# The inversion of the routing slots by pairs of token columns

## The chip, the cores and the metric

The kernel runs on one core of a Trainium2 chip. The core has five engines that work side by side: TensorE (matrix products, PE in the rows, with its weight loads as PEld), VectorE (DVE), ScalarE (ACT), GpSimd (POOL) and SyncE (SP, which here issues transfers). They meet by semaphores. The metric is the time on the device in microseconds. A difference of about 0.2% is what a comparison of two such kernels can tell from none.

## The reference

Three stages follow one another: a recurrent attention, a feed-forward layer with a leaky activation, and a layer of eight experts in which each expert takes exactly N / E = 384 of the N = 3072 tokens.

```python
def _moe2_ref(x, w_gate, w1, w2):
    cap = N // E
    logits = x @ w_gate
    order = np.argsort(-logits.flatten())
    for idx in order:                      # tokens go to their best expert that has room
        tok, e = idx // E, idx % E
        if assigned[tok] >= 0 or counts[e] >= cap:
            continue
        assigned[tok] = e
        counts[e] += 1
    for e in range(E):
        mask = assigned == e
        out[mask] = np.maximum(x[mask] @ w1[e], 0.0) @ w2[e]
```

## The kernel before

Attention and the first layer fill the time up to about 540 us. What matters here is the rest: eight rounds, one for each expert in the order in which the experts fill up. A round p has a routing part, which finds the expert that fills next and the 384 tokens it gets, and a feed-forward part (two layers, 384 -> 1024 -> 384, each fp32 product made of three fp32r products, `product3`). The routing of round p runs beside the feed-forward part of round p - 1, except in round 0, where nothing runs beside it.

The tokens lie on 128 partitions in NT = 24 columns. The routing part of a round is a chain between VectorE and TensorE:

- a search with six steps: VectorE makes a grid (`grid`, bf16), TensorE counts it (`count_pair`: two token columns at a time, so 12 products of 128 stationary and 16 moving columns), VectorE compares, TensorE turns the result into a digit;
- `close`, `slots`: which tokens belong to the expert, and a slot number from 1 to 384 for each (0 for the others);
- the inversion: from "token has slot s" to "slot s holds token t". VectorE splits the slot into `place` (64 values) and `col` (6 values), and marks them: `is_b` is 128 x 24 x 64 (fp16, 1 where the place fits; made in two halves of 12 columns, `inversion_b`), and `is_ar` is 128 x 24 x 6 (the token's row number where the column fits). TensorE (`inverse`) sums over all tokens: 24 products, one for each token column j, with `is_b[:, j]` (64 columns) stationary and `is_ar[:, j]` (6 columns) moving, all into 64 x 6 values of `banks[7]`. Each half has 12 of them;
- `indices`: VectorE adds N / 2 and writes the row numbers as integers to `idx`, two operations of 64 x 3. GpSimd's gather waits for them (`xg`, three indirect copies a round), TensorE transposes the gathered rows (`turn_rows`), ScalarE and VectorE split them (`xeh`, `xel`).

Where TensorE does the routing's products inside the stream of the feed-forward part is written out by hand in `body(new)`: a body has 48 places, at each stands one triple of large products (three of 128 x 384), and tables say at which place a count, a digit, the offsets, a half of the inversion or a transpose goes in ahead of the triple. The two halves of the inversion stand at places 44 and 45 (round 1), 40 and 41 (round 2), 38 and 39 (rounds 3 to 6), 25 and 26 (round 7). In round 0 they follow one another. What stands in the stream between two triples is called a break below.

VectorE's order is written out too (`route`): after `inversion_b` come `relu_lo(p - 1, 3)` (the low part of a hidden tile of the expert before, `gl` in the rows), `front_best` (the best logit of each token for the next round, ending with the `onehot` of 128 x 192), `indices`, `front_rank`, `relu_lo(p - 1, 4)`, the keys, `survivors`, and the first grid of the next round.

Of the kernel before, what the change touches and what calls it, by code (L numbers as in the profile page):

```python
# [13 lines left out]
ALU = mybir.AluOpType  # L14
# [3 lines left out]
P = 128  # L18
HALF = 64
# [13 lines left out]
def build(nc, rT, kT, rN, kN, v, wT, uR, w_in, w_out, alpha, w_gate, w1, w2, out):  # L33
# [3 lines left out]
    E, _, F2 = w1.shape  # L37
    KD = DM // P
    NF, NF2 = F // P, F2 // P
    NT = NCH * B  # L40
    N = NT * P
    CAP = N // E
    NA = CAP // P
    NS = CAP // HALF
# [5 lines left out]
    with ExitStack() as ctx:  # L50
        def sb(name, shape, dt=F32, scope=ctx):
            return scope.enter_context(nc.sbuf_tensor(name, shape, dt))

        def sem(name):
            return ctx.enter_context(nc.semaphore(name))

        banks = [ctx.enter_context(nc.psum_tensor(f"bank{i}", [P, 512], F32)) for i in range(8)]
# [54 lines left out]
        q = sb("q", [P, 2, TB], F32, one)  # L112
# [18 lines left out]
        is_b = sb("is_b", [P, NT, HALF], FP16)  # L131
        is_a = sb("is_a", [P, NT, NS])
        is_ar = sb("is_ar", [P, NT, NS], FP16)
# [30 lines left out]
        idx = sb("idx", [P, E, NA], I32)  # L164
        xeh = sb("xeh", [P, 2, KD, CAP], F32R)
        xel = sb("xel", [P, 2, KD, CAP], F32R)
        last_gh = sb("last_gh", [P, CAP], F32R)
        last_gl = sb("last_gl", [P, CAP], F32R)


        consts_loaded, u_loaded, wcol_set = sem("consts_loaded"), sem("u_loaded"), sem("wcol_set")
# [27 lines left out]
        expert_ready, idx_ready = sem("expert_ready"), sem("idx_ready")  # L199
# [35 lines left out]
        def halves(j):  # L235

            return slice(j * HALF, j * HALF + HALF)
# [560 lines left out]
        def _(dve):  # L798
# [134 lines left out]
            V = nc.vector  # L933
# [215 lines left out]
            def indices(p):  # L1149

                dve.wait_ge(inverse_done, p + 1)
                parts = banks[7][0:HALF, 0:NS].rearrange("p (a u) -> p u a", u=2)
                for u in range(2):
                    V.tensor_scalar(idx[halves(u), p], parts[:, u], float(N // 2), None, ALU.add).then_inc(idx_ready, 1)

            def while_counting(p, m):

# [135 lines left out]
            inversion_b(E - 1)  # L1293
            relu_lo(E - 2, 0)
            indices(E - 1)
            for f in range(1, 6):
                relu_lo(E - 2, f)
# [9 lines left out]
        def _(pe):  # L1307
# [151 lines left out]
            def busy(n, bank):  # L1459
                for _ in range(n):  # L1460
                    nc.tensor.matmul(bank[:, 0:TB], idle_b[:, 0:P], idle_b[:], start=True, stop=True, skip_group_check=True)
# [4 lines left out]
            for h in range(H):  # L1466
                for j in range(2):
                    mm = nc.tensor.matmul(banks[7][halves(j), h * D:(h + 1) * D], down[0:D, h], ident[0:D, 0:D],
                                          start=(h == 0), stop=(h == H - 1), skip_group_check=True)
# [38 lines left out]
            def count(p, m):  # L1508
                if m == 1:
                    pe.wait_ge(onehot_ready, p + 1)  # L1510
                if p > 0:
                    pe.wait_ge(grid_ready, 2 * V3 * (p + 1) + m)
                elif m == 1:
                    pe.wait_ge(grid_ready, 2)
                for i in range(KNOWN // 2 if p == 0 and m == 1 else 0, NT // 2):
                    if p == 0 and m > 1 and i % (NT // 4) == 0:
                        pe.wait_ge(grid_ready, 2 * m - (1 if i == 0 else 0))
                    mm = count_pair(i)
                mm.then_inc(counts_done, 1)
# [11 lines left out]
            for b in range(B):  # L1531
                for k in range(KD):
                    mm = nc.tensor.matmul(banks[7][:, b * E:(b + 1) * E], x2T[:, k, b * P:(b + 1) * P], wg[:, k],
                                          start=(b == 0 and k == 0), stop=(b == B - 1 and k == KD - 1), skip_group_check=True)
# [14 lines left out]
            def digit(p, m):  # L1549
                level, n = divmod(m - 1, V3)  # L1550
                pe.wait_ge(hits_ready, p * 2 * V3 + m)
                nc.tensor.matmul(full_at[level], sized[0:BASE_ROW + 1, level, n], hits[0:BASE_ROW + 1], start=(n == 0), stop=True, skip_group_check=True).then_inc(digit_ready, 1)

            def offsets(p):
                pe.wait_ge(running_ready, p + 1)
                nc.tensor.matmul(banks[5][:, 0:2], before_b[:], running[:].rearrange("p (s j) -> p s j", s=2)[:, :, NT - 1], start=True, stop=False, skip_group_check=True)
                nc.tensor.matmul(banks[5][:, 1:2], after_b[:], running[:, NT - 1:NT], start=False, stop=True, skip_group_check=True).then_inc(offsets_done, 1)

            def inverse(p, half):
                pe.wait_ge(inverse_ready, 3 * p + 1 + half)  # L1560
                if p == 0 and half == 0:
                    pe.wait_ge(rows_numbered, 1)
                for j in range(half * NT // 2, (half + 1) * NT // 2):
                    mm = nc.tensor.matmul(banks[7][0:HALF, 0:NS], is_b[:, j], is_ar[:, j], start=(j == 0), stop=(j == NT - 1))  # L1564
                if half == 1:
                    mm.then_inc(inverse_done, 1)

            def turn_rows(p, a):

                pe.wait_ge(gathered[a], 16 * (p + 1))  # L1570
                if a > 0 and p >= 1:
                    pe.wait_ge(xgl_ready, NA * p + a)
                for k in range(KD):
                    mm = nc.tensor.transpose(turned_rows(p, a)[:, k], xg[:, a, k * P:(k + 1) * P], ident)
                mm.then_inc(xgt_done, 1)
# [25 lines left out]
            def stream(s):  # L1601

                p, at = divmod(s, 6 * NF2)
                pair, which = divmod(at, 3)
                if pair == 0:
                    if p < E:
                        expert_hidden(p, 0, which)
                elif pair == 1:
                    if p >= 1:
                        expert_back(p - 1, NF2 - 1, which)  # L1610
                elif pair % 2 == 0:
                    expert_hidden(p, pair // 2, which)
                else:
                    expert_back(p, pair // 2 - 1, which)

            def body(new):

                q = new + 1
                counts_at = ((2, 5, 18, 23, 27, 31), (7, 11, 15, 19, 23, 27), (3, 7, 12, 17, 21, 25))[new] if new < 3 else (2, 7, 11, 16, 21, 25)
                digits_at = ((4, 6, 19, 24, 28, 32), (9, 13, 16, 20, 24, 28), (5, 10, 14, 18, 22, 26))[new] if new < 3 else (4, 9, 13, 17, 22, 26)  # L1620
                offsets_at = (36, 32)[new] if new < 2 else 30
                inverses_at = ((44, 45), (40, 41))[new] if new < 2 else (38, 39) if new < E - 2 else (25, 26)
                turns_at = ((4, 4, 5), (9, 11, 13), (7, 9, 11))[new] if new < 3 else (5, 7, 10)
                busy_at = {0: 9, 2: 2, 4: 4, 5: 2, 6: 1, 7: 1} if new == 0 else {}
                for at in range(6 * NF2):
                    if q < E - 1:
                        for m in range(2 * V3):
                            if at == counts_at[m]:
                                count(q, m + 1)
                            if at == digits_at[m]:  # L1630
                                digit(q, m + 1)
                        if at == offsets_at:
                            offsets(q)
                        if at in inverses_at:
                            inverse(q, inverses_at.index(at))
                    elif q == E - 1:
                        if at == 2:
                            offsets(q)
                        if at in inverses_at:
                            inverse(q, inverses_at.index(at))  # L1640
                    for a in range(NA):
                        if at == turns_at[a]:
                            turn_rows(new, a)
                    busy(busy_at.get(at, 0), banks[0])
                    while done[0] < 6 * NF2 * new + at + 1 - BEGINS:
                        stream(done[0])
                        done[0] += 1
# [4 lines left out]
            for m in range(1, 2 * V3 + 1):  # L1652
                count(0, m)
                digit(0, m)
                if m in (1, 2):
                    last_rows(m + 1)
            offsets(0)
            inverse(0, 0)
            inverse(0, 1)
            for p in range(E):  # L1660
                body(p)
# [38 lines left out]
```

## Time and profile before

| | |
|---|---|
| median of 3 runs | 809.49 us (808.98 to 809.88) |
| span of the profiled execution | 808.1 us, its only time on the page |
| TensorE busy | 770.3 us, 95% |
| VectorE busy | 500.5 us, 62% |
| GpSimd busy | 474.9 us, 59% |
| ScalarE busy | 220.1 us, 27% |

The span is the time from the first to the last instruction of one profiled execution; the runs are timed apart, without the profiler. TensorE's busy time is not a measure of its work, since products overlap. So the start of a product is the reliable number, and what one break takes is read from the starts around it.

### The profile page before, as it was taken

The numbers are of one execution on the slowest core, as the hardware profiler recorded it, in microseconds if no ns is written. First come the engines' busy times: TensorE is split into PE (matmuls) and PEld (weight loads), VectorE is DVE, ScalarE is ACT, GpSimd is POOL, SyncE is SP. The second block draws the span as 40 slices with busy tenths as digits, with TensorE's granted clock in tenths as the row PEclk, the third lists the DMA queues.
The fourth block names the chain that finished last, engine by engine and source line by source line (L and its number), as shares of the span: only waits on it lengthen the run. The fifth ranks groups of instructions, "written<-read, shape, count | busy, mean of one in ns | idle before, by whom it ended". The sixth has DMA issues, their size and how long they took to land.

```text
span 808.1 us, 15970 instructions
## 1 busy us (share of the span) xinstructions
PE 770.3 (95%) x6320; PEld 649.6 (80%) x6320; DVE 500.5 (62%) x1038; ACT 220.1 (27%) x452; POOL 474.9 (59%) x471
## 2 busy tenths in 40 slices
PE   6899999999999999999999999939999999999997
PEld 4578888888888888888888888726887988989996
DVE  8877766556655565556655334477787777776221
ACT  1233322111211121112111211204244344353451
POOL 6899985555555555555554333107477775775871
PEclk8999999999999999999999999958999999999999
DMA  7865522222221222222000000014523605517401
GB/s 213 228 197 155 150 70 70 69 69 70 67 67 63 66 67 63 64 64 67 11 11 11 11 11 10 14 54 168 186 74 144 215 20 198 171 45 272 159 11 49
DMA packets 46569, 75.17 MB, mean 93 GB/s; under 512 B 6256, under 2 KB 31856, under 8 KB 46496
## 3 DMA queue, kind: packets, MB, share of 16 engines
q1 hardware_dynamic: 37776, 56.07, 22.1%
q10 hardware_dynamic: 5584, 8.46, 3.7%
q0 software_dynamic: 3136, 9.64, 3.4%
q8 instruction: 50, 0.82, 0.5%
q14 instruction: 23, 0.19, 0.1%
HBM read 64.71 MB, written 9.44 MB: 92 GB/s over the span
## 4 chain that ended last, share of the span: by engine, by line
PE 81%; DVE 11%; POOL 2%; issue 2%; ACT 2%; DMA 1%; SPq 0%; POOLq 0%; DVEq 0%; ACTq 0%
PE bank L1312 23%; PE bank L1314 22%; PE bank L1313 21%; PE bank L1329 3%; PE bank L1363 3%; PE bank L1346 2%; DVE grid L1205 2%; PE bank L1422 2%; PE bank L1505 2%; DVE grid L1203 1%; POOL gl L493 1%; PE bank L1564 1%; DVE both L860 1%; PE bank L1382 1%; DVE xel L1120 1%
## 5 line engine op out<-in xcount | busy, mean ns | idle before, releaser
L493 POOL TENSOR_TENSOR gl<-g,gh 128x512 fp32r<-128x512 f32 x96 | 128.2, 1336 | 202.4 <-ACT gh L667 202.2
L1003 DVE TENSOR_SCALAR q<-bank,alpha_sb 128x512 f32<-128x512 f32 x96 | 71.9, 749 | 146.2 <-PE bank L1314 146.0
L667 ACT CAST gh<-g 128x512 fp32r<-128x512 f32 x96 | 59.6, 621 | 335.4 <-PE bank L1314 298.8
L1312 PE MATMUL bank<-gh,wout_h 128*128 128x512 f32 x288 | 118.7, 412 | 1.2 <-DVE vs L887 0.4
L1312 PE MATMUL bank<-xTh,win_h 128*128 128x512 f32 x288 | 113.1, 393 | 0.3 <-DVE xTl L896 0.3
L1314 PE MATMUL bank<-gh,wout_l 128*128 128x512 f32 x288 | 112.8, 392 | 0.0
L1313 PE MATMUL bank<-gl,wout_h 128*128 128x512 f32 x288 | 112.4, 390 | 0.0
L1314 PE MATMUL bank<-xTh,win_l 128*128 128x512 f32 x288 | 112.2, 389 | 0.0
L1313 PE MATMUL bank<-xTl,win_h 128*128 128x512 f32 x288 | 112.0, 389 | 0.0
L599 POOL TENSOR_TENSOR w1l<-raw,w1h 128x384 fp32r<-128x384 f32 x64 | 65.1, 1016 | 38.4 <-ACT w2h L731 37.9
L1312 PE MATMUL bank<-xeh,w1h 128*128 128x384 f32 x192 | 69.6, 362 | 0.0
L1006 DVE SCALAR_TENSOR_TENSOR g<-bank,q 128x512 f32<-128x512 f32 x96 | 66.4, 691 | 3.3
L1312 PE MATMUL bank<-w2h,gh 128*128 128x384 f32 x189 | 68.0, 360 | 0.1
L1312 PEld LDWEIGHTS bank<-gh,wout_h 128*128 128x128 f32 x288 | 54.1, 188 | 14.7 <-POOL gl L493 2.6
L600 POOL TENSOR_TENSOR w2l<-raw,w2h 128x384 fp32r<-128x384 f32 x64 | 64.9, 1015 | 0.0
L1314 PE MATMUL bank<-xeh,w1l 128*128 128x384 f32 x192 | 64.7, 337 | 0.0
L1313 PE MATMUL bank<-xel,w1h 128*128 128x384 f32 x192 | 64.4, 336 | 0.0
L1313 PE MATMUL bank<-w2l,gh 128*128 128x384 f32 x189 | 63.8, 338 | 0.0
L1314 PEld LDWEIGHTS bank<-gh,wout_l 128*128 128x128 f32 x288 | 54.0, 188 | 12.1
L1314 PE MATMUL bank<-w2h,gl 128*128 128x384 f32 x189 | 63.7, 337 | 0.0
L1312 PEld LDWEIGHTS bank<-xTh,win_h 128*128 128x128 f32 x288 | 54.1, 188 | 11.8 <-DVE xTl L896 0.8
L1314 PEld LDWEIGHTS bank<-xTh,win_l 128*128 128x128 f32 x288 | 54.1, 188 | 11.5
(203 smaller groups left out, 1453.6 us busy)
## 6 DMA issues: line engine op xcount, KB each, us to landing
raw<-w SPq DMA_DIRECT2D x32, 768.0 KB
rt<-rT SPq DMA_DIRECT2D x48, 96.0 KB, 2.9
vs<-v SPq DMA_DIRECT2D x48, 96.0 KB, 3.0
vn<-v SPq DMA_DIRECT2D x24, 192.0 KB, 2.9
x2rows<-x2n SPq DMA_DIRECT2D x23, 192.0 KB, 1.9
kt<-kT SPq DMA_DIRECT2D x44, 96.0 KB, 2.5
kn<-kN SPq DMA_DIRECT2D x20, 192.0 KB, 2.5
rn<-rN SPq DMA_DIRECT2D x20, 192.0 KB, 2.6
```

The source lines that it names most:

```text
L493: nc.gpsimd.tensor_tensor(gl[:, f % 2], g[:, f % 2], gh[:, f % 2].bitcast(F32), ALU.subtract).then_inc(gl_ready, 1)
L599: nc.gpsimd.tensor_tensor(w1l[:, f], raw1[:, p % 2, :, f * P:(f + 1) * P], w1h[:, f].bitcast(F32), ALU.subtract).then_inc(wlo1_ready, 1)
L600: nc.gpsimd.tensor_tensor(w2l[:, f], raw2[:, p % 2, f, :], w2h[:, f].bitcast(F32), ALU.subtract).then_inc(wlo_ready, 1)
L667: nc.scalar.copy(gh[:, f % 2], g[:, f % 2]).then_inc(gh_ready, 1)
L1003: nc.vector.tensor_scalar(q[:, f % 2], h, 0.0, alpha_sb[:, f:f + 1], ALU.min, ALU.mult).then_inc(q_ready, 1)
L1006: nc.vector.scalar_tensor_tensor(out=g[:, f % 2], in0=h, scalar=0.0, in1=q[:, f % 2], op0=ALU.max, op1=ALU.add).then_inc(g_ready, 1)
L1205: V.scalar_tensor_tensor(out=grid[:, js, 0:R], in0=wide, scalar=found[level], in1=row, op0=ALU.subtract, op1=ALU.is_ge).then_inc(grid_read ...
L1312: nc.tensor.matmul(o, a_h, b_h, start=first, stop=False)
L1313: nc.tensor.matmul(o, a_h, b_l, start=False, stop=False)
L1314: return nc.tensor.matmul(o, a_l, b_h, start=False, stop=last)
L1329: mm = nc.tensor.matmul(score_bank(c, b, j)[halves(j), h * HT:(h + 1) * HT], kt[heads_in(j), b % 2, h], weights(c, b)[heads_in(j), j, h], ...
L1363: return nc.tensor.matmul(y_bank(c, b)[halves(j), cols], weights(c, b)[:, j, h], vs[:, b, j, cols], start=(h == 0), stop=(h == H - 1), ski ...
```

## The change

The inversion takes two token columns at a time. The stationary operand is `is_b` of columns 2i and 2i + 1 side by side (128 columns), the moving one is `is_ar` of the same two (12 columns), and 12 products give 128 x 12 values. Of their four blocks the two diagonal ones are wanted: rows 0 to 63 with columns 0 to 5 (even token columns), and rows 64 to 127 with columns 6 to 11 (odd ones). VectorE adds N / 2 to the second and writes it to a new tile, `odd_rows`, in partitions 0 to 63, waits until that is written, and then adds the two blocks into `idx`, again in two operations. TensorE does all 12 products at one place, the later of the two; it still waits for the first half of `is_b` ahead of the first six and for the second half ahead of the others.

```diff
+        odd_rows = sb("odd_rows", [P, NS])
...
                 dve.wait_ge(inverse_done, p + 1)
-                parts = banks[7][0:HALF, 0:NS].rearrange("p (a u) -> p u a", u=2)
+                inv_hold(V.tensor_scalar(odd_rows[0:HALF], banks[7][halves(1), NS:2 * NS], float(N // 2), None, ALU.add))
+                even, odd = (a.rearrange("p (a u) -> p u a", u=2) for a in (banks[7][0:HALF, 0:NS], odd_rows[0:HALF]))
                 for u in range(2):
-                    V.tensor_scalar(idx[halves(u), p], parts[:, u], float(N // 2), None, ALU.add).then_inc(idx_ready, 1)
+                    V.tensor_tensor(idx[halves(u), p], even[:, u], odd[:, u], ALU.add).then_inc(idx_ready, 1)
...
                 pe.wait_ge(inverse_ready, 3 * p + 1 + half)
                 if p == 0 and half == 0:
                     pe.wait_ge(rows_numbered, 1)
-                for j in range(half * NT // 2, (half + 1) * NT // 2):
-                    mm = nc.tensor.matmul(banks[7][0:HALF, 0:NS], is_b[:, j], is_ar[:, j], start=(j == 0), stop=(j == NT - 1))
+                for i in range(half * NT // 4, (half + 1) * NT // 4):
+                    mm = nc.tensor.matmul(banks[7][:, 0:2 * NS], is_b[:, 2 * i:2 * i + 2].rearrange("p j s -> p (j s)"),
+                                          is_ar[:, 2 * i:2 * i + 2].rearrange("p j s -> p (j s)"), start=(i == 0), stop=(i == NT // 2 - 1))
...
-                inverses_at = ((44, 45), (40, 41))[new] if new < 2 else (38, 39) if new < E - 2 else (25, 26)
+                inverse_at = (45, 41)[new] if new < 2 else 39 if new < E - 2 else 26
...
-                        if at in inverses_at:
-                            inverse(q, inverses_at.index(at))
+                        if at == inverse_at:
+                            inverse(q, 0)
+                            inverse(q, 1)
```

On TensorE, in the stream of round 3's inversion, the order before is this (each row one product, L1564 the inversion, the others the triples):

```order
L1312 MATMUL bank<-w2h,gh 128x384
L1313 MATMUL bank<-w2l,gh 128x384
L1314 MATMUL bank<-w2h,gl 128x384
L1564 MATMUL bank<-is_ar,is_b 64x6 x12
L1312 MATMUL bank<-w2h,gh 128x384
L1313 MATMUL bank<-w2l,gh 128x384
L1314 MATMUL bank<-w2h,gl 128x384
L1564 MATMUL bank<-is_ar,is_b 64x6 x12
L1312 MATMUL bank<-xeh,w1h 128x384
L1313 MATMUL bank<-xel,w1h 128x384
L1314 MATMUL bank<-xeh,w1l 128x384
```

and at the same place of the changed kernel (its lines are numbered two higher there):

```order
L1314 MATMUL bank<-w2h,gh 128x384
L1315 MATMUL bank<-w2l,gh 128x384
L1316 MATMUL bank<-w2h,gl 128x384
L1314 MATMUL bank<-w2h,gh 128x384
L1315 MATMUL bank<-w2l,gh 128x384
L1316 MATMUL bank<-w2h,gl 128x384
L1566 MATMUL bank<-is_ar,is_b 128x12 x12
L1314 MATMUL bank<-xeh,w1h 128x384
L1315 MATMUL bank<-xel,w1h 128x384
L1316 MATMUL bank<-xeh,w1l 128x384
```

One break is gone, and the triple that stood between the two now comes ahead of both halves.

On VectorE, behind the making of `is_b` in a round from 3 on, before:

```order
L1147 TENSOR_TENSOR is_b<-iota_b,bank 128x768 x2
L1113 SCALAR_TENSOR_TENSOR gl<-bank,gh 128x384
L956 TENSOR_REDUCE bank<-logits 128x24
L957 TENSOR_TENSOR onehot<-logits,bank 128x192
L1154 TENSOR_SCALAR idx<-bank 64x3 x2
L961 TENSOR_TENSOR ranked<-onehot,bank 128x192
L962 TENSOR_REDUCE bank<-ranked 128x24
L1113 SCALAR_TENSOR_TENSOR gl<-bank,gh 128x384
L970 TENSOR_TENSOR onehot<-ranked,bank 128x192
```

and after the change (lines one or two higher):

```order
L1148 TENSOR_TENSOR is_b<-iota_b,bank 128x768 x2
L1114 SCALAR_TENSOR_TENSOR gl<-bank,gh 128x384
L957 TENSOR_REDUCE bank<-logits 128x24
L958 TENSOR_TENSOR onehot<-logits,bank 128x192
L1153 TENSOR_SCALAR odd_rows<-bank 64x6
L1156 TENSOR_TENSOR idx<-bank,odd_rows 64x3 x2
L962 TENSOR_TENSOR ranked<-onehot,bank 128x192
L963 TENSOR_REDUCE bank<-ranked 128x24
L1114 SCALAR_TENSOR_TENSOR gl<-bank,gh 128x384
L971 TENSOR_TENSOR onehot<-ranked,bank 128x192
```

The operation on `odd_rows` is new, ahead of the indices, and nothing else has moved.

## Rows read from the trace of the kernel before

**Rows 1.** The page: span, and the chain that ended last by engine.

```profile
span 808.1 us, 15970 instructions
...
PE 81%; DVE 11%; POOL 2%; issue 2%; ACT 2%; DMA 1%; SPq 0%; POOLq 0%; DVEq 0%; ACTq 0%
```

**Rows 2.** Busy: stage, us, PE, PEld, DVE, ACT, POOL, clock, DMA share, GB/s.

```profile
668.50:700.00 31.50, 31.27 (x259) 28.07 (x258) 24.41 (x71) 13.31 (x30) 21.55 (x22) 1.00 0.39 132
790.00:800.00 10.00, 10.00 (x60) 10.00 (x59) 2.23 (x4) 1.94 (x5) 0.00 (x0) 1.00 0.00 0
```

**Rows 3.** Timeline, TensorE, one old break: start us, us, engine, line, work, [idle].

```profile
636.23 0.34 PE L1314 MATMUL bank<-w2h,gl 128*128 128x384 f32 x1
...
636.49 0.45 PEld L1564 LDWEIGHTS bank<-is_ar,is_b 128*64 128x64 f16 x12 [0.25 <-DVE is_b L1147]
...
636.97 0.45 PE L1312 MATMUL bank<-w2h,gh 128*128 128x384 f32 x1
...
637.25 0.33 PE L1313 MATMUL bank<-w2l,gh 128*128 128x384 f32 x1
```

**Rows 4.** The same view, one break for a count.

```profile
643.87 0.34 PE L1314 MATMUL bank<-w2h,gl 128*128 128x384 f32 x1
...
644.04 0.37 PEld L1505 LDWEIGHTS bank<-onehot,grid 128*128 128x128 bf16 x12 [0.16 <-issue]
...
644.36 0.42 PE L1312 MATMUL bank<-w2h,gh 128*128 128x384 f32 x1
...
644.62 0.33 PE L1313 MATMUL bank<-w2l,gh 128*128 128x384 f32 x1
```

**Rows 5.** Timeline, VectorE: a small operation with a PSUM and an SBUF input.

```profile
644.74 0.16 DVE L1211 TENSOR_TENSOR hits<-bank,rest 40x8 bf16<-40x8 f32 x1
```

**Rows 6.** Timeline, VectorE, round 3: from is_b to the next grid.

```profile
635.27 1.81 DVE L1147 TENSOR_TENSOR is_b<-iota_b,bank 128x768 f16<-128x768 bf16 x2
...
637.85 0.35 DVE L957 TENSOR_TENSOR onehot<-logits,bank 128x192 f32<-128x192 f32 x1
638.34 0.34 DVE L1154 TENSOR_SCALAR idx<-bank 64x3 int32<-64x3 f32 x2
...
639.10 0.36 DVE L962 TENSOR_REDUCE bank<-ranked 128x24 f32<-128x192 f32 x1
...
640.63 0.56 DVE L1113 SCALAR_TENSOR_TENSOR gl<-bank,gh 128x384 fp32r<-128x384 f32 x1 [1.17 <-issue]
...
642.74 1.15 DVE L1203 TENSOR_TENSOR grid<-key,bank 128x960 bf16<-128x960 f32 x1
```

**Rows 7.** Timeline, VectorE and TensorE, round 1.

```profile
573.48 0.35 DVE L957 TENSOR_TENSOR onehot<-logits,bank 128x192 f32<-128x192 f32 x1
...
574.73 0.34 DVE L1154 TENSOR_SCALAR idx<-bank 64x3 int32<-64x3 f32 x2 [0.90 <-PE bank L1564]
...
576.50 0.19 PEld L1312 LDWEIGHTS bank<-w2h,gh 128*128 128x128 f32 x1 [0.43 <-DVE gl L1113]
```

**Rows 8.** Timeline, VectorE and TensorE, round 2.

```profile
602.75 1.81 DVE L1147 TENSOR_TENSOR is_b<-iota_b,bank 128x768 f16<-128x768 bf16 x2
...
603.75 0.45 PEld L1564 LDWEIGHTS bank<-is_ar,is_b 128*64 128x64 f16 x12 [0.24 <-DVE is_b L1147]
...
606.91 0.34 DVE L1154 TENSOR_SCALAR idx<-bank 64x3 int32<-64x3 f32 x2 [1.57 <-PE bank L1564]
...
611.49 0.45 PE L1505 MATMUL bank<-onehot,grid 128*128 128x16 bf16 x12 [0.52 <-DVE grid L1203]
```

**Rows 9.** Round 3's last gather, its landing, and its transposes.

```profile
641.50 0.95 POOL L589 DMA_INDIRECT xg<-x2rows,idx  x1 [0.30 <-issue]
...
DMA to landing us min/median/max: 5.7/5.7/5.7
...
649.95 0.49 PE L1574 MATMUL bank<-id_wg,xg 128*128 128x128 f32 x3
```

**Rows 10.** Timeline, VectorE, round 0: the indices.

```profile
546.41 0.34 DVE L1154 TENSOR_SCALAR idx<-bank 64x3 int32<-64x3 f32 x2 [0.18 <-PE bank L1564]
```

## What the change should do to the time

> **What bounds the kernel now.** I read the page first, then the busy time by stage, then the timelines of TensorE and VectorE around one inversion. The span is 808.1 us, and 81% of the chain that ended last is TensorE [rows 1]. In the part that the change touches (routing beside the expert FFN) TensorE is busy 31.27 of 31.50 us in a round; after the last inversion it is busy 10.00 of 10.00 us, at a granted clock of 1.00, the 2.4 GHz level [rows 2]. The last ten microseconds of the kernel then follow TensorE's last product. So a microsecond that TensorE saves in any of rounds 1 to 7 should come off the end, unless some wait takes its place. In those 10.00 us 59 weight loads start, 0.17 us each: that is the pace of the undisturbed stream of fp32r products.
>
> **What two breaks cost.** Today each round puts two packets of 12 small products into the stream. From the last large product before a packet to the second one after it there are 636.23 to 637.25 = 1.02 us [rows 3]. Two undisturbed steps of 0.174 take 0.35, so one break costs 0.67 us, two cost 1.34. The trace has the shape of the new break already: a count is 12 products of 128 stationary and 16 moving bf16 columns. Measured the same way, 643.87 to 644.62 = 0.75 us, it costs 0.40 [rows 4]. It is cheaper although it loads twice the columns: its 12 weight loads span 0.37 us against 0.45, it starts 0.16 us behind the load before it against 0.25, and the stream resumes 0.32 us after its first load against 0.48. The new inversion differs from it in fp16 for bf16 and 12 moving columns for 16. I take 0.40 for it. Saved: 1.34 - 0.40 = 0.94 us a round.
>
> The new break's cost isn't measured at fp16, so bounds: from below, 12 loads at the count's spacing without entry or exit, about 0.3 us; from above, 12 steps at the pace of the fp32r stream, 12 x 0.17 = 2.1 us, plus the count's 0.1 of entry and exit, 2.2. I take the value of the count, the nearest row by far.
>
> The Trainium skill ("TensorE: Matmul & The Clock Gate", section "LDWEIGHTS (loading the stationary operand)") has a weight load cost by its columns alone, P/1.2 ns. By its figure, an estimate, the new packet would take 12 x 0.107 = 1.28 us and the old ones 24 x 0.053, the same, so that the change would bring next to nothing; as a mechanism of this kernel that is rival A. The rows above disagree for bf16: twice the columns took less time. The same page's section "Weight-path perf modes — Fast Weight Load (FWL) and DoubleRow" lets the fast load apply to 128 weights of any type but fp32, which would carry the count's cost over to fp16, and the sum with it; no row of before has fp16 at 128 columns.
>
> **What the merge waits for.** Both halves now stand at the later of the two places, so that the second half of is_b has less time. In round 3, is_b is done at 635.27 + 1.81 = 637.08 [rows 6]. After the change three products follow the one at 636.23, the break starts about 636.92, and its seventh product would come at 637.07; is_b's signal needs some 0.05, so TensorE waits about 0.05 there. The same pattern stands in rounds 4 to 6. In round 2 is_b ends at 602.75 + 1.81 = 604.56, while TensorE, which started its old first break at 603.75 [rows 8], would want the seventh product near 603.49 + 0.70 + 0.15 = 604.34: a wait of 0.28. Rounds 1 and 7 have is_b in time.
>
> **What VectorE gets.** One more operation, the odd rows plus N/2 from PSUM to SBUF, and a wait until it is written; the two index operations turn from one-input into two-input. An operation with PSUM and SBUF inputs on 40 x 8 took 0.16 us [rows 5], and the two index operations of before 0.34 together, so 0.19 for each with its start [rows 6]. I take 0.21 for the new one and nothing for the other two. Bounds: 0.16, the operation without a gap behind it, and 0.6 if the two index operations also double. Queued behind it on VectorE are the rank, relu_lo 4, the keys and the first grid of the next round, and on GpSimd the gather.
>
> Where does that lie? In round 3, front_best ends at 637.85 + 0.35 = 638.20 and the first index operation starts at 638.34. After the change TensorE's break ends before that, so VectorE starts at about 638.26, is 0.21 longer, and ends the indices near 638.80, 0.12 later in absolute time, although TensorE is 0.89 earlier. VectorE reaches the end of the rank at 639.46 now, then 639.6. It waits there until 640.63 for relu_lo 4's input, an idle of 1.17 us, which TensorE and ScalarE set; that input comes 0.89 earlier, at 639.74. So the cover of 1.17 shrinks to about 0.15 but holds, and from relu_lo 4 to the grid (642.74 to 643.89) and the count that takes it (644.04, with 0.16 of idle as any count has) everything moves by 0.89 with TensorE [rows 4, 6].
>
> The gather has more cover. The third copy is issued at 641.50 and lands 5.7 us later, at 647.2; its transposes stand at 649.95 [rows 9]. Copies are issued 0.1 later and wanted 0.9 earlier: 1.7 us of the 2.7 are left. I saw no wait for a gather in the waits of TensorE, the first copy has less room, and if it were late, it is a few tenths.
>
> **Rounds 0, 1, 2.** In round 0 nothing covers the chain. VectorE waits 0.18 us for the old inversion [rows 10]; half as many products end before front_best does, which gives 0.15, and the new operation takes 0.21: 0.06 slower. In round 1 the path runs through VectorE: the indices start 0.90 us late, at 574.73, because of the inversion, and TensorE then waits 0.43 at 576.50 for relu_lo 4 behind them [rows 7]. After the change front_best's end, 573.48 + 0.35 = 573.83, decides: the start is at 573.88, 0.85 earlier, less 0.21, so the round gains 0.64 instead of 0.94. In round 2 the indices started at 606.91, 1.57 us idle, long after TensorE's break, and the first count then waited (0.52 us idle on TensorE) for the grid [rows 8]. I can't say what held them; I take it to stay as it is relative to TensorE: 0.94 - 0.28 = 0.66. If it goes away, the round gains 0.6 more; if it stays at its absolute time, the round gives up its 0.66 and 0.21 besides.
>
> **Sum.** Round 1 0.64, round 2 0.66, rounds 3 to 6 4 x 0.89 = 3.56, round 7 0.94 (VectorE has nothing urgent there), round 0 -0.06: 5.74 us. The profiled span of 808.1 us becomes 802.4. The median of the runs is 809.49, 1.4 above that span; I take these 1.4 to stay: 803.7 us.
>
> **Rivals.**
> A. The new break isn't as cheap as a count: loads of 128 fp16 columns paced by their columns. The old break's 12 loads in 0.45 us are 0.0375 each, 128 columns would be 0.075, against 0.37 / 12 = 0.031 in the count: 0.53 us more a round than I count, 3.7 in rounds 1 to 7: 807.4. For it: fp16 at this width isn't in the trace. Against: the count's rows. Chance 0.08.
> B. VectorE takes over (the slower side). Its chain from is_b over front_best, the indices, rank, keys and grid to the first count is then tied to VectorE's own pace, TensorE waits there for whatever it saved, and the 0.21 is paid in each of rounds 1 to 6 and in round 0: about 1.5 us slower less round 7's 0.94 and some slack of 0.09 a round; with index operations near 0.3 each it is 0.45 a round, +2.7 - 0.9 = +1.8, 811.3. It decides once VectorE's cover of 1.17 us at relu_lo 4 is used up, that is from 0.15 us more than I count in each round. For it: the grid ends 0.15 us before its count begins even now. Against: that cover is idle time on VectorE, in the rows. Chance 0.05.
> C. Half of it: some rounds give back what they gained, at the first count or at the first gathered rows (the first copy goes out behind the weight load). Two or three of the rounds lost would leave 3 us: 806.5. Chance 0.12.
> D. No change measurable: B's wait eats the gain, without a loss: 809.0. Chance 0.06.
> E. Round 2's late indices go as well: 0.6 more, 803.1; inside the forecast's own spread.
> The forecast with E has 0.69.
>
> The measurement tells about 0.2% (1.6 us) from no change. Faster by more than that: the forecast, A, C: 0.89. Within: D and part of B: 0.07. Slower: 0.04. The range: low 802.3, if round 2 loses its stall and the break costs 0.1 less; high 807.5, which takes in A and C.
>
> **What would show it.** The 12 products of the inversion in one group with 128x12, its loads spanning about 0.37 us and the large product resuming 0.32 us after the first; TensorE's start-to-start over it 0.75 us; is_b named as releaser inside the break in round 2 only, by 0.3; odd_rows 0.16 us and the two idx operations 0.34; the idle before relu_lo 4 in round 3 down from 1.17 to 0.15; the first count of a round still at 0.16 of idle; a round of 30.7 us where it is 31.6 now. I am wrong if the group's loads span 0.6 us or more, or if counts or transposes at the start of a round show waits of half a microsecond for the grid or for xg.

## The result

The changed kernel took 806.58 us (median of 6 runs, 804.67 to 807.45) against 809.31 (808.98 to 809.88) of the kernel before: a ratio of 0.9965, 95% interval 0.9955 to 0.9974. That is 2.7 us faster where 5.7 were forecast. The profiled execution has a span of 805.7 us against 808.1, and its run took 807.45, the slowest of the six. A second profile, of e9 below, has a span of 803.1.

The page of the changed kernel, the chain that ended last by engine:

```profile
span 805.7 us, 15778 instructions
...
PE 77%; DVE 13%; DMA 4%; issue 2%; ACT 2%; POOL 1%; another core or an unknown queue 0%; SPq 0%; POOLq 0%; DVEq 0%; ACTq 0%
```

TensorE's share fell from 81% [rows 1], and VectorE and the DMA have taken it up. Half of the DMA's 4% is the gather (`xg`, 2% of the span by line), which the chain before did not contain.

The new break, in the timeline of the changed kernel (start us, length us, engine, line, work, idle ahead), round 1:

```profile
574.34 0.34 PE L1316 MATMUL bank<-w2h,gl 128*128 128x384 f32 x1
574.51 0.37 PEld L1566 LDWEIGHTS bank<-is_ar,is_b 128*128 128x128 f16 x12 [0.16 <-issue]
...
574.83 0.42 PE L1314 MATMUL bank<-xeh,w1h 128*128 128x384 f32 x1
...
575.09 0.34 PE L1315 MATMUL bank<-xel,w1h 128*128 128x384 f32 x1
```

From the last large product ahead to the second behind it: 574.34 to 575.09 = 0.75 us, the count's figure to the hundredth [rows 4], where one of the two old breaks had 1.02 [rows 3]. The loads span 0.37 us with 0.16 of idle ahead. Less two undisturbed steps of 0.35 us together, the new break costs 0.40 in rounds 1 and 7; it costs 0.45 in rounds 3 to 6 and 0.68 in round 2, where TensorE waits in it for the second half of `is_b`.

VectorE in round 3, the rows that answer to [rows 6]:

```profile
638.77 0.17 DVE L1153 TENSOR_SCALAR odd_rows<-bank 64x6 f32<-64x6 f32 x1
638.97 0.34 DVE L1156 TENSOR_TENSOR idx<-bank,odd_rows 64x3 int32<-64x3 f32 x2
...
640.27 0.56 DVE L1114 SCALAR_TENSOR_TENSOR gl<-bank,gh 128x384 fp32r<-128x384 f32 x1 [0.18 <-ACT gh L738]
```

The new operation takes 0.17, its successor starts 0.20 after its start, and the two index operations still take 0.34. The idle time ahead of relu_lo 4 is 0.18, where it was 1.17. The first count of the next round has its usual idle:

```profile
643.68 0.37 PEld L1507 LDWEIGHTS bank<-onehot,grid 128*128 128x128 bf16 x12 [0.16 <-issue]
```

All of this is as forecast. What was not stands in two other places. First, TensorE waits for the gathered rows. In rounds 5 and 6 (the transposes of the first 128 rows):

```profile
707.84 0.31 PEld L1577 LDWEIGHTS bank<-id_wg,xg 128*128 128x128 f32 x3 [0.49 <-DMA xg<-x2rows,idx]
...
739.04 0.31 PEld L1577 LDWEIGHTS bank<-id_wg,xg 128*128 128x128 f32 x3 [1.00 <-DMA xg<-x2rows,idx]
```

In rounds 1 and 4 the same wait is 0.55 and 0.38 us.

Second, TensorE's clock rises later in round 0. Busy time by stage, one microsecond of the changed kernel (stage, us, PE, PEld, DVE, ACT, POOL, granted clock, DMA share, GB/s):

```profile
552.00:553.00 1.00, 1.00 (x6) 1.00 (x6) 0.96 (x2) 1.00 (x3) 1.00 (x2) 0.50 0.11 40
```

and the same of the kernel before:

```profile
552.00:553.00 1.00, 1.00 (x8) 0.64 (x7) 0.96 (x2) 1.00 (x4) 1.00 (x2) 1.00 0.05 18
```

Before, the granted clock rises to 1.00 (the 2.4 GHz level) at about 550.5 us, after the change at about 554.3. The first product of the expert stream starts at 556.55 instead of 555.34, 1.21 us later, although the inversion of round 0 starts at the same moment in both (544.65 and 544.64).

Set side by side product by product (the hidden products of the same number in both traces), the changed kernel is 1.21 us behind at the first, level in round 2 (-0.06), 0.33 ahead after round 3's inversion, 1.22 after round 4's, 1.80, 2.35 and 2.39 after those of rounds 5, 6 and 7. Each inversion brings about 0.9; 0.26, 0.37 and 0.89 go again at the transposes behind the inversions of rounds 4, 5 and 6; 1.1 goes at one place in round 2.

### The profile page after: what moved, and what is told of

Read it like the earlier page. It is cut to its first block, busy times and chain, and to the rows that moved or that the text cites. A ratio compares the mean times of both kernels' runs of the same rounds, so it can differ in the third digit from the quotient of the medians.

```text
span 805.7 us, 15778 instructions
## 1 busy us (share of the span) xinstructions
PE 762.4 (95%) x6216; PEld 645.1 (80%) x6224; DVE 502.1 (62%) x1046; ACT 220.7 (27%) x452; POOL 475.3 (59%) x471
## 4 chain that ended last, share of the span: by engine, by line
PE 77%; DVE 13%; DMA 4%; issue 2%; ACT 2%; POOL 1%; another core or an unknown queue 0%; SPq 0%; POOLq 0%; DVEq 0%; ACTq 0%
PE bank L1314 22%; PE bank L1316 20%; PE bank L1315 20%; PE bank L1331 3%; PE bank L1365 3%; DMA xg<-x2rows,idx 2%; PE bank L1348 2%; DVE grid L1207 2%; PE bank L1424 2%; PE bank L1507 2%; DVE grid L1205 1%; PE bank L1577 1%; DVE both L861 1%; PE bank L1384 1%; DVE is_b L1148 1%
```

## The experiments

Every kernel was timed against the kernel before on one chip: e1 to e4 on a first, e5 to e8 on a second, e9 to e12 on a third. Times are compared within such a group, and across groups only by the ratios. Ratios have their 95% interval behind them; 0.001 is 0.8 us. Each kernel has one profile, of one execution.

**e1, fillers in round 0** of the changed kernel:

```diff
             inverse(0, 0)
+            busy(1, banks[0])
             inverse(0, 1)
+            busy(1, banks[0])
```

> The changed kernel, with one filler product (bf16, 128 x 512) between the two halves of round 0's inversion and one more behind the second half, so that TensorE has no pause between 544.6 and 550. Theory 1 (the 12 wide products leave TensorE less busy in round 0, and the granted clock rises one step later, at 554.1 instead of 550.5 us): the clock is at 2.4 GHz by about 551 again, the first product of the expert stream starts near 555.4 instead of 556.55, and the kernel is 1.2 us faster than the changed one, 805.4 us or 4.0 under the one before. Rival (the clock rises in its own time, whatever this stretch does): no shift of the first product in a consistent direction, 806.6.

Measured: 0.9952 (0.9939 to 0.9966), 804.18 us against 808.24. The clock rises at about 550.1, and the first expert product comes 10.57 us behind the first product of round 0's inversion (10.70 before, 11.90 in the changed kernel). The distance is shown by the trace. That the time follows is likely by size (1.1 us better than the changed kernel by the ratios, 1.2 expected), though the two intervals overlap.

**e2, wide products at the two old places** (the table `inverses_at` of before, `inverse` as changed).

> The changed kernel's 12 wide products, but six at each of the two old places. If a break's cost is mostly entry and exit, each of the two costs about 0.25 us, 0.5 together, and the rounds 1 to 7 save 0.84 each less what they give back: nearly all of the gain remains, within 1 us of the changed kernel. If the gain is in having one break only, two breaks of 0.4 cost 0.8 us a round, and 2.8 us of the gain are lost: as slow as the kernel before.

Measured: 0.9962 (0.9949 to 0.9976). The break of six, in round 1:

```profile
573.24 0.34 PE L1316 MATMUL bank<-w2h,gl 128*128 128x384 f32 x1
573.42 0.31 PE L1566 MATMUL bank<-is_ar,is_b 128*128 128x12 f16 x6
...
573.84 0.34 PE L1315 MATMUL bank<-w2l,gh 128*128 128x384 f32 x1
```

0.60 us, less 0.35 for two undisturbed steps, is 0.25 for each. So two wide breaks cost 0.50 in rounds 1 and 7, where one costs 0.40. In rounds 3 to 6 they cost 0.50 against 0.45, and in round 2, which waits for `is_b` either way, 0.68 against 0.68. Nearly all of the gain is in the wide form (twice the columns, half as many products), and with it the merge brings 0.1 us a round at most. The clock is late here too (553.5; first expert product 11.71 behind).

**e3, narrow products in one break**, the converse: `inverse` as before, both halves at the later place.

> The kernel before with its 24 narrow products in one break at the later place, and no new VectorE operation. From the old break (0.67 us for 12, its loads 0.45) one break of 24 should take about 1.1 us, against 1.34 for two: 0.2 us a round saved, 1.6 us at most in all, 807.7. If the narrow loads alone are the price (24 x 0.0375 = 0.9 us and no entry), 0.4 a round, 806.5.

Measured: 0.9976 (0.9966 to 0.9986), 1.9 us faster, a little more than the first case. The break in round 3:

```profile
634.50 0.34 PE L1314 MATMUL bank<-w2h,gl 128*128 128x384 f32 x1
634.77 0.92 PE L1564 MATMUL bank<-is_ar,is_b 128*64 128x6 f16 x24
...
635.91 0.33 PE L1313 MATMUL bank<-xel,w1h 128*128 128x384 f32 x1
```

1.41 - 0.35 = 1.06 us against 1.34 for two, in every one of the rounds 1 to 7. A round gains 0.3, and keeps it: no wait for a gather shows.

**e4, one more VectorE operation** in the kernel before:

```diff
                 dve.wait_ge(inverse_done, p + 1)
+                inv_hold(V.tensor_scalar(odd_rows[0:HALF], banks[7][0:HALF, 0:NS], float(N // 2), None, ALU.add))
```

> The kernel before with one more VectorE operation of 64 x 6 ahead of the two index operations of each round, waited for, its result unused. It adds 0.21 us to the chain behind the inversion in every round. If VectorE's chain bounded the rounds: 7 x 0.21 = 1.5 us slower, 810.8. If its idle time covers it except in rounds 0, 1 and 2: 0.2 to 0.6 us slower, 809.5 to 809.9, not to be told from none.

Measured: 1.0002 (0.9993 to 1.0011). VectorE's chain has room for 0.2 us in the kernel before: the idle ahead of relu_lo 4 falls from 1.17 to 0.97 us in rounds 3 to 6, and nothing behind it moves (in round 1, where VectorE is in the path [rows 7], the stream loses 0.2). This doesn't yet test rival B, whose condition is the smaller cover that is left once TensorE has moved.

**e5, wide in round 0 alone**, rounds 1 to 7 as before (`if p == 0` around the new products and index operations).

> The kernel before, with the wide products and the new VectorE operation in round 0 alone; rounds 1 to 7 as before. Theory 1 (fewer and shorter products in round 0 make the granted clock rise one step, some 3 to 4 us, later): the clock is still at its lower level at 551 to 553 us, the first product of the expert stream starts about 1.1 us later against round 0's first inversion product than before (11.8 us behind it where it is 10.7 before), and the kernel is about 1.2 us slower than before. Rival (no influence of round 0): within 0.3 us of before.

Measured: 1.0014 (1.0005 to 1.0024), 1.3 us slower than before. The clock is at 0.50 until 553.7, the first expert product 12.20 us behind the first inversion product. In this execution the clock also fell back to 0.50 between about 560.5 and 564, which the others don't show, and the stream lost 1.4 us more there. How many of the eleven runs did so isn't known, so the 1.3 us can't be put down to the late rise alone.

**e6, weights behind the gather**, on the changed kernel:

```diff
-                    if p == 0 and c == 1:
+                    if p < E - 1 and c == 1:
                         for a in range(NA):
-                            sp.wait_ge(gathered[a], 16)
+                            sp.wait_ge(gathered[a], 16 * (p + 1))
```

> The changed kernel, with the second half of each expert's weights loaded only once the gather of the same round has landed (in rounds 1 to 6, as round 0 does already). Theory 2 (TensorE's waits of 0.4 to 1.0 us for the gathered rows in rounds 1, 4, 5 and 6 come from the gather queueing behind the weight load): these waits vanish, and so does most of ScalarE's wait for the first half of the weights; 1.1 to 1.5 us faster than the changed kernel. Rival (the gather's own time sets its landing, with or without the load beside it): the waits stay, 806.6. If the second half comes too late instead, ScalarE waits for it at its fifth piece and the kernel gets slower.

Measured: 0.9947 (0.9934 to 0.9961), 1.5 us better than the changed kernel by the ratios, as expected, though the intervals overlap. No transpose waits for the gather any more. ScalarE's waits for the first half of the weights stayed (0.9 to 1.7 us in rounds 3 to 6), a miss in the expectation that cost nothing. The second half came late once: ScalarE waited 1.31 us for it at 744.57, and TensorE 0.30 us behind that at 748.19.

**e7, e1 and e6 together.**

> Both edits on the changed kernel: the two fillers of round 0 and the weights' second half behind the gather. If the two causes are apart, their gains add: 1.2 and 1.1 to 1.5 us less than the changed kernel, a ratio to before near 0.993, so 5.5 us under it, about what the forecast had.

Measured: 0.9942 (0.9929 to 0.9956), 4.5 us under before instead of 5.5, and only 0.7 under e6: in these runs the two gains did not add. Its profile has the early clock and no wait for the gather, but ScalarE's late start in round 2, of which more below, 1.1 us at that place.

**e8, later transposes** on e1: `turns_at` (6, 8, 11) instead of (5, 7, 10) in rounds from 3 on.

> The changed kernel with the fillers of round 0, and in rounds from 3 on the transposes of the gathered rows at places 6, 8 and 11 where they stand at 5, 7 and 10. Theory 2: TensorE's waits for the gather in rounds 4 to 6, 0.2 to 0.7 us each, shrink by about 0.5 each, 0.5 to 1.0 us faster than with the fillers alone, unless the last rows then come late for the first hidden product. Rival: what TensorE waits for there is the chain behind it, and the same wait shows at the next place.

Measured: 0.9997 (0.9988 to 1.0006), 3.6 us slower than e1 by the ratios: a clear miss. VectorE takes the work in a written order, and the split of the gathered rows (`rows_lo`) stands ahead of the routing's next step. A later transpose delays that step, and TensorE waits at the count:

```profile
647.95 0.56 DVE L1121 TENSOR_TENSOR xel<-bank,xeh 128x384 fp32r<-128x384 f32 x1 [0.84 <-ACT xeh L744]
...
648.42 0.17 DVE L1216 TENSOR_REDUCE bank<-bank 128x1 f32<-128x8 f32 x1
...
649.90 0.37 PEld L1507 LDWEIGHTS bank<-onehot,grid 128*128 128x128 bf16 x12 [1.12 <-DVE grid L1207]
```

The reduction could have started at 647.95, when its digit was done, but xel was ahead of it and waited for ScalarE. The waits for the first rows did shrink, to between 0.11 and 0.38 us in rounds 3, 5 and 6, as theory 2 had it; what neither expectation had is the new and larger wait at the count.

**e9, the changed kernel once more.**

> The changed kernel once more, on the same chip as the three that follow, with a second profile. The clock in round 0 rises late again (after 553 us, or it falls back before 554), the first expert product comes 11.7 to 12.2 us behind round 0's first inversion product, TensorE waits for the gather in two or more of the rounds 1 and 4 to 6, and the ratio to before is 0.9965 within 0.001. Open: whether ScalarE's late start in round 2 (2.96 us idle ahead of one gh) shows again, or belongs to single executions.

Measured: 0.9963 (0.9949 to 0.9976). The clock rises after 553, the first expert product is 11.85 us behind; the waits for the first rows, ahead of their weight load, are 0.74, 0.56 and 1.06 us in rounds 1, 5 and 6. ScalarE's late start in round 2 did not show.

**e10, round 0 as before, rounds 1 to 7 changed.**

> The changed kernel, but round 0 as in the kernel before (24 narrow products, no added VectorE operation). Theory 1: the first expert product comes 10.5 to 10.8 us behind the first inversion product, as with the fillers, and the kernel is 1.2 us faster than the changed one. Rival: the fillers of the first experiment helped for another reason than the clock, and nothing changes here.

Measured: 0.9950 (0.9936 to 0.9963), 804.46 us (803.70 to 805.01) against 805.49 (804.19 to 806.34) of e9, which ran on the same chip: 1.0 us where 1.2 was expected. The first expert product comes 10.54 us behind. Waits for the gather are still there, in rounds 3, 5 and 6.

**e11, e10 with the weights behind the gather.**

> The same, with the weights' second half behind the gather in rounds 1 to 6. No wait of TensorE for the gather, the early clock: about 0.8 us under the kernel of e10, 4.6 to 5.5 us under the kernel before, the fastest of the study or level with the one of e7.

Measured: 0.9928 (0.9914 to 0.9941), 802.74 us (802.16 to 803.47) against 808.47: 5.7 us faster than the kernel before, and the fastest of the study. It is 1.7 us faster than e10, with no overlap of the runs, where 0.8 was expected; the profile of e10 loses 0.44, 0.53 and 0.74 us at the transposes behind the inversions of rounds 3, 5 and 6, 1.7 together, and that of e11 nothing. This is the clearest measure of what the gather costs. That 5.7 is also the forecast's figure is in part chance, since round 2 brings 1.3 us here and not the 0.66 of the forecast. The gather's landing, from issue, in the changed kernel's round 5:

```profile
DMA to landing us min/median/max: 5.8/5.8/5.8
```

and in the same round of e11:

```profile
DMA to landing us min/median/max: 3.0/3.1/3.2
```

**e12, three operations on `odd_rows`** in the kernel of e1.

> The kernel with the fillers of round 0 and the VectorE operation on odd_rows done three times, each waited for: 0.42 us more in the chain behind each inversion. If VectorE's cover ahead of relu_lo 4 is nearly used up (0.15 us left by the forecast), rounds 3 to 6 each lose about 0.27 at the first count, and rounds 4 to 6 as much again at the gather where that waits: 1.1 to 2.5 us slower than with the fillers alone. If there is still cover, as in e4 (0.2 us for one more operation in the kernel before), less than 0.6.

Measured: 0.9980 (0.9970 to 0.9990), 2.3 us slower than e1 by the ratios. In its profile the clock rose at about 547, fell back at 550.4 and rose again at 553.8, and round 0 alone is 1.7 us longer than in e1; the wait for round 6's first rows grew to 1.30. The idle ahead of relu_lo 4 is gone in rounds 3 to 6, and TensorE has 0.39 us of idle ahead of the next first count in rounds 3 to 5 instead of 0.16. Round 3 gained 0.85 at its inversion and gave back 0.24 at that count (-1.26 to -1.02, product by product), rounds 4 and 5 the same, which no other kernel did; rounds 1 and 2 gained 0.4 less each than in e1. So VectorE's cover is used up by 0.4 us more, as forecast, and rounds 1 to 5 of this profile pay 1.5 us for it. How the 2.3 us of the medians divide between this and the clock the single profile doesn't tell.

## Why the prediction was right, and where it was off

The sign, the mechanism and the range were right (802.3 to 807.5 holds 806.58); the gain was half of the figure. That it stayed inside the range is partly luck: the clock of round 0, which took 1.2 us, stood in no rival. Step by step:

1. *The cost of the breaks.* Right: 0.40 for the new one as measured in the count, 1.34 for the two old ones. The rule of the Trainium skill that has a load cost P/1.2 ns by its columns ("TensorE: Matmul & The Clock Gate", "LDWEIGHTS (loading the stationary operand)") didn't hold for this: 12 loads of 128 fp16 columns span 0.37 us, 12 of 64 had 0.45. The Trainium skill's rule on the same page for the fast load at 128 weights of a type other than fp32 ("Weight-path perf modes — Fast Weight Load (FWL) and DoubleRow") agrees with the fp16 row. Rival A is out. e2 and e3 split the gain, 0.94 a round: 0.28 from one break instead of two while the products are narrow, 0.66 from the wide form; with wide products the second break costs only 0.10. From the four measured breaks one can estimate what lies behind this: six more wide products add 0.40 - 0.25 = 0.15 us, 0.025 each, so that 0.10 is left for going in and out; twelve more narrow ones add 1.06 - 0.67 = 0.39, 0.033 each, and 0.28 is left. By this estimate 0.28 of the narrow break's 0.67 is entry and exit.
2. *The wait for is_b* within the merged break: in round 3 the loads span 0.42 instead of 0.37, the 0.05 of the forecast, and in round 2 the break costs 0.68 instead of 0.40, its 0.28.
3. *VectorE.* 0.20 for the new operation (0.21 forecast), nothing for the others, cover of 0.18 left (0.15), no wait at the first count. Rival B did not come, and e12 shows how near it was: with three times the operation the cover is gone and the first counts wait.
4. *The gather.* This step failed. It was argued on the third copy, which had 2.7 us of room and has 1.2 to 3.0 left in rounds 3 to 6 (1.7 by the forecast); the wait is on the first copy, whose room wasn't worked out, and it was put at "a few tenths". In e3, which has 0.3 of the gain, the first copy lands only 0.9 to 1.1 us ahead of its transposes in rounds 3 to 6. In the changed kernel TensorE's wait was 0.4 to 1.1 us ahead of the transposes' weight load, and the stream lost 0.26 + 0.37 + 0.89 = 1.5 us in rounds 4 to 6 of the first profile, 0.44 + 0.93 = 1.4 in rounds 5 and 6 of the second. The prediction's own sign of being wrong, transposes that wait half a microsecond for `xg`, was there. In round 1 the wait of the first profile takes 0.63 us, which is made up soon after, since in the kernel before a count waits for its grid there. The reason is what TensorE's earlier start did not move: the gather shares the DMA with the next expert's weights, whose load begins ahead of the breaks and so keeps its time, while the transposes come 0.9 us earlier. e6 and e11 show it: with half of the weights behind the gather, the copies of round 5 land 3.1 us after issue instead of 5.8, and the waits are gone. It agrees with the Trainium skill ("Trainium Kernel Development and Optimization", "Key Constraints"), by which transfers issued from different queues run on the same 16 DMA engines and interleave. This is rival C (chance 0.12), with its place at the gathered rows.
5. *Round 0.* This step was mis-sized, and its reason was missed: 0.06 us by the chain of VectorE, 1.15 to 1.21 by the clock. The chain was right: idx starts at 546.48 where it was 546.41. But TensorE had 24 products in 1.66 us there, and has 12 in two groups of 0.33 with 0.54 idle between them; the kernel's filler products behind them (L1463, products without a use, there to keep TensorE busy) start and end about 0.6 us earlier, and the pause ahead of the first count is 0.89 us instead of 0.25. In the changed kernel the clock then stays at its lower level (1.2 GHz) for 3.8 us more. The chain that ended last shows what that does. In the kernel before it runs in this stretch through the weights' load and ScalarE, beside which TensorE's work finds room (start us, us, what):

```profile
543.06 6.44 DMA raw<-w
...
552.93 0.38 ACT xeh L743
```

After the change it runs through TensorE itself from 550.59 to 555.40, counts, transposes and fillers:

```profile
550.59 0.47 PE bank L1507 x12
...
551.93 1.38 PE bank L1577 x6
553.31 1.41 PE bank L1463 x4
```

A filler starts 0.43 us after the one ahead of it at the lower level and 0.22 at the upper one (e12), and 2.3 us of this chain are fillers. e5 alone makes the kernel slower, by a ratio of 1.0014; e1, e10 and e11 bring the early rise back. By profile, from the first inversion product to the first expert product:

| narrow, or with fillers | us | wide, no fillers | us |
|---|---|---|---|
| before | 10.70 | changed | 11.90 |
| e1 | 10.57 | e2 | 11.71 |
| e3 | 10.47 | e5 | 12.20 |
| e4 | 10.68 | e6 | 12.21 |
| e7, e8 | 10.75, 10.74 | e9 | 11.85 |
| e10, e11 | 10.54, 10.62 | | |

The one exception is e12, with fillers and 12.28. There and in e6 the clock rises early (at 547.0 and 547.4) and falls again (at 550.4 and 550.9), behind a pause of TensorE that lasted until the first count (1.92 and 1.44 us). So the fillers make the early rise likely, not certain, and what exactly sets the moment of the rise these profiles don't show.

6. *Rounds 1 and 2.* Round 1 was forecast at 0.64 and gained 0.63 in e9 (0.07 behind at its start, 0.56 ahead after its inversion and relu_lo 4) and 0.67 in e1. Round 2, 0.66 with a surplus of 0.6 if the late indices went away: in e1, e9 and e10 they did, and it gained 1.3. In the first profile something else was late instead, ScalarE at one tile:

```profile
611.93 0.49 ACT L738 ACTIVATE gh<-bank 128x384 fp32r<-128x384 f32 x1 [2.96 <-remote]
...
612.45 0.56 DVE L1114 SCALAR_TENSOR_TENSOR gl<-bank,gh 128x384 fp32r<-128x384 f32 x1 [1.73 <-ACT gh L738]
```

It took 1.1 us from the stream. The same instruction is as late in the profiles of e5 to e8, and not in e1 to e4 nor e9 to e12. The changed kernel has it in one profile and not in another, so it is not the kernel alone that decides it. It may be the single execution, or the chip: e5 to e8 ran on one chip and the others on two more, and e7, which by the ratios is 1.1 us slower than e11, ran on that one. What holds ScalarE there is open, and so is what held the indices at 606.91 before [rows 8].

The sum with the measured terms, for e9: rounds 1 to 7 brought 0.63 + 1.31 + 0.86 + 0.93 + 0.87 + 0.89 + 0.9, together 6.4, the clock took 1.15 and the gather 1.4; it comes to 3.9, plus 1.1 us by which that execution reached round 0 earlier, and its span is 5.0 us shorter than that of before. The medians' 3.0 (e9) and 2.7 lie below 3.9 (e9's profiled run is 0.6 us below its own median); executions of the changed kernel vary by 2.8 us, those of before by 0.9, and the two slowest of the changed one's six have the lowest mean clock (0.973 and 0.974, the fastest 0.978). How often the other executions carry ScalarE's late start can't be said from single profiles.

## What to carry to other kernels

Small products in a stream cost by their number and by each entry and exit: where two token columns could share one stationary operand of 128 columns, half as many loads took less time than the narrow ones, even though two of the four blocks of each result are not used. When work is taken out of the bounding engine, list what does not move with it (here the weight load that the gather shares the DMA with) and compare the first thing wanted, not the last. And work that an engine did in a stretch where it waits anyway may have brought its clock up: look at the granted clock ahead of the next stretch before taking it away.

## What the runs showed of the hardware

- 12 loads of 128 fp16 columns span 0.37 us and enter with 0.16 of idle; 12 of 64 columns span 0.45 and enter with 0.25.
- The clock can rise and fall again within a few microseconds: in e6 it had risen at 547.4, TensorE then idled for 1.44 us ahead of the count at 549.58, and the clock was at 0.50 again from 550.9 to 554.3.
- A break in the stream of large products costs 0.25 us with 6 products of 128 stationary columns, 0.40 with 12 of them, 0.67 with 12 of 64 columns and 1.06 with 24 of these (e2, changed kernel, before, e3).
- Three indirect copies of 128 rows land 5.8 us after issue beside weights still under way, 3.1 us with half of those weights put behind them (round 5 of the changed kernel and of e11).
